# A buffer of its own for the fourth tile's rows, and its transposes ahead of half an output product

## The reference, cut to what matters

```python
def _moe2_ref(x, w_gate, w_local, w1, w2):
    logits = np.einsum('bsd,de->bse', x, w_gate)
    local_gate = 1.0 / (1.0 + np.exp(-np.einsum('bsd,de->bse', x, w_local).squeeze(-1)))
    for b in range(B):
        prev_e = -1
        for s in range(S):
            fresh_e = int(np.argmax(logits[b, s]))
            if s == 0 or local_gate[b, s] < 0.5:
                e = fresh_e
            else:
                e = prev_e if prev_e >= 0 else fresh_e
            prev_e = e
            ...                      # p = softmax(logits[b, s])
            h = np.maximum(x[b, s] @ w1[e], 0.0)     # w1[e]: 512 x 1024
            out[b, s] = p[e] * (h @ w2[e])           # w2[e]: 1024 x 512
```

## Time and profile before

| | |
|---|---|
| median of three runs | 755.41 us |
| profiled execution, its own time | 755.69 us |
| its span | 754.0 us |
| granted clock of PE, mean over the span | 0.994 |
| PE busy | 737.2 us, 98% |
| DVE, ACT, POOL busy | 299.8, 230.8, 143.0 us |
| HBM read, written | 48.79 MB, 10.31 MB |

### The profile page before, as it was taken

One profiled execution on the slowest core, in us unless ns is written; L12 is line 12 of the kernel. 1 busy time (PEld: TensorE's weight loads), 2 busy tenths in 40 slices (PEclk: granted clock), 3 DMA queues, 4 the chain that ended last, 5 costly groups with the idle time before them and its releaser, 6 DMA issues.

```text
span 754.0 us, 13862 instructions
## 1 busy us (share of the span) xinstructions
PE 737.2 (98%) x4756; PEld 672.6 (89%) x4757; DVE 299.8 (40%) x620; ACT 230.8 (31%) x435; POOL 143.0 (19%) x164
## 2 busy tenths in 40 slices
PE   6999999999999999999999999999899999999997
PEld 5879999999999999999999999888688888888885
DVE  6546241226241216241214732595534562222531
ACT  3753133114133114133113024222524462222531
POOL 7472020002020002020000015102313141211221
PEclk9999999999999999999999999999999999999999
DMA  9930314001304001300001340103832653101000
GB/s 222 384 77 15 80 30 98 1 2 49 78 27 102 1 1 45 83 15 18 1 1 37 112 157 2 57 23 105 334 114 71 216 196 110 50 28 50 30 24 12
DMA packets 71995, 57.62 MB, mean 76 GB/s; under 512 B 54892, under 2 KB 57228, under 8 KB 71952
## 3 DMA queue, kind: packets, MB, share of 16 engines
q1 hardware_dynamic: 68432, 47.58, 21.0%
q0 software_dynamic: 3520, 9.44, 3.7%
HBM read 48.79 MB, written 10.31 MB: 78 GB/s over the span
## 4 chain that ended last, share of the span: by engine, by line
PE 93%; DMA 2%; ACT 2%; DVE 1%; issue 1%; POOL 0%; SPq 0%; DVEq 0%; POOLq 0%; ACTq 0%
PE bank L606 41%; PE bank L727 15%; PE bank L752 14%; PE bank L548 4%; PE bank L577 4%; PE bank L739 2%; PE bank L519 2%; PE bank L616 2%; PE bank L571 2%; PE bank L627 2%; PE bank L675 1%; PE bank L536 1%; PE bank L558 1%; ACT wc_h L962 1%; DMA kraw<-in_k_dram 1%
## 5 line engine op out<-in xcount | busy, mean ns | idle before, releaser
L606 PE MATMUL bank<-u_h,wc_h 128*128 128x288 f32 x384 | 119.5, 311 | 0.0
L606 PE MATMUL bank<-hid_h,wc_h 128*128 128x288 f32 x384 | 117.0, 305 | 0.0
L727 PE MATMUL bank<-wslots,xgT_h 128*128 (+1 forms) x344 | 111.9, 407 | 1.6 <-DVE xgT_l L1367 1.6
L606 PE MATMUL bank<-hid_l,wc_h 128*128 128x288 f32 x384 | 113.3, 295 | 0.0
L606 PE MATMUL bank<-u_l,wc_h 128*128 128x288 f32 x384 | 113.1, 295 | 0.0
L606 PE MATMUL bank<-u_h,wc_l 128*128 128x288 f32 x384 | 113.1, 294 | 0.0
L606 PE MATMUL bank<-hid_h,wc_l 128*128 128x288 f32 x384 | 113.1, 294 | 0.0
L752 PE MATMUL bank<-wslots,hT_h 128*128 (+1 forms) x336 | 104.0, 391 | 0.0
L1376 DVE SCALAR_TENSOR_TENSOR hid_l<-bank,hid_h 128x288 fp32r<-128x288 f32 x96 | 43.4, 454 | 125.3 <-ACT hid_h L919 124.7
L919 ACT ACTIVATE hid_h<-bank 128x288 fp32r<-128x288 f32 x96 | 39.3, 409 | 117.4 <-PE bank L606 117.4
L727 PEld LDWEIGHTS bank<-wslots,xgT_h 128*128 128x128 f32 x344 | 62.0, 190 | 14.1 <-issue 2.2
(11 more groups left out here) (260 smaller groups left out, 1061.2 us busy)
## 6 DMA issues: line engine op xcount, KB each, us to landing
w1raw<-in_moe_w_dram SPq DMA_DIRECT2D x20, 512.0 KB, 3.6
w2raw<-in_moe_w_dram SPq DMA_DIRECT2D x20, 512.0 KB, 5.3
wc_raw<-in_moe_w_ch_dram SPq DMA_DIRECT2D x8, 768.0 KB, 10.1
x_rows<-x1n SPq DMA_DIRECT2D x16, 256.0 KB, 2.2
kb<-in_k_dram SPq DMA_DIRECT2D x24, 128.0 KB, 3.0
qb<-in_q_dram SPq DMA_DIRECT2D x24, 128.0 KB, 2.9
vb_e<-in_v_dram SPq DMA_DIRECT2D x16, 128.0 KB, 3.0
vb_o<-in_v_dram SPq DMA_DIRECT2D x16, 128.0 KB, 3.0
```

The source lines that it names most:

```text
L606: last = pe.matmul(to, lhsT, rhs, start=(m == 0), stop=(m == len(mms) - 1))
L727: last = pe.matmul(bank[half][:, :], xgT[a][:, c, :], w1s[x][:, bass.ds(n & 1, 1), c, half * 512:(half + 1) * 512].rearrange("p a n -> p ( ...
```

## The change

The fourth tile (tile 3) gets a row buffer `xg3`, an id buffer `id_in3` and a semaphore `x3_in` of its own. POOL clears `xg3` once, ahead of gather(0), beside the clearing of `xg`. The loop over the first three tiles in POOL's program is written out: gather(2), scatter(0), the waits for x1 and `routed` 1, gather(3) into `xg3`, a wait for `xgT_ready` 3 (that is `x_turn(2)`), gather(4) into `xg`, scatter(1), scatter(2). PE's `x_turn(3)` reads `xg3`, and stands ahead of the second six products of `output(2, 0, 0)` instead of behind them. SP waits for `x3_in` and for four gathers on `x_in`. A tensor `end_of_rows` only keeps a stretch of SBUF free, so that `xg3` lies behind it.

```diff
--- before.py
+++ after.py
@@ -181,6 +181,7 @@
             prob_t = sb(part2, "prob_t", [P, NT])
             id_in = sb(part2, "id_in", [P, 1], I32)
             id_out = sb(part2, "id_out", [P, 1], I32)
+            id_in3 = sb(part2, "id_in3", [P, 1], I32)
 
 
             table = sb(part2, "table", [1, NTP], I32)
@@ -234,6 +235,8 @@
             loads_f = sb(part2, "loads_f", [1, E])
             loads = sb(part2, "loads", [1, 2, E], I32)
             yo = sb(part2, "yo", [P, D])
+            sb(part2, "end_of_rows", [P, 1128])
+            xg3 = sb(part2, "xg3", [P, D])
 
         w1s = [wslots[:, :, x, :].rearrange("p s (c f) -> p s c f", c=KD) for x in range(2)]
         w2s = [wslots[:, :, 2 + x, :].rearrange("p s (c d) -> p s c d", c=KF) for x in range(2)]
@@ -272,7 +275,7 @@
 
         raw_in = [sem(f"raw_in{i}") for i in range(NU)]
         w_hi, w_split = sem("w_hi"), sem("w_split")
-        id_in_set, id_out_set, x_in = sem("id_in_set"), sem("id_out_set"), sem("x_in")
+        id_in_set, id_out_set, x_in, x3_in = sem("id_in_set"), sem("id_out_set"), sem("x_in"), sem("x3_in")
         rows_asked, rows_given = sem("rows_asked"), sem("rows_given")
         xgT_ready, xgT_hi, xgT_done = sem("xgT_ready"), sem("xgT_hi"), sem("xgT_done")
         h_ready, hs_done, hT_ready, hT_hi, hT_done = sem("h_ready"), sem("hs_done"), sem("hT_ready"), sem("hT_hi"), sem("hT_done")
@@ -478,7 +481,8 @@
                         load_unit(e, i)
 
             sp.wait_ge(versions_known, 1)
-            sp.wait_ge(x_in, 16 * (EARLY + 2))
+            sp.wait_ge(x3_in, 16)
+            sp.wait_ge(x_in, 16 * (EARLY + 1))
             for n in range(1, E):
                 load_weights(n)
 
@@ -670,9 +674,15 @@
                     x_turn(0)
 
             def x_turn(t):
-                pe.wait_ge(x_in, 16 * (t + 1))
+
+                of_routed = isinstance(t, int) and t == EARLY
+                if of_routed:
+                    pe.wait_ge(x3_in, 16)
+                else:
+                    pe.wait_ge(x_in, 16 * (t + 1) if isinstance(t, int) else 16 * t)
+                rows_in = xg3 if of_routed else xg
                 for c in range(KD):
-                    last = pe.transpose(bank[4][:, c * P:(c + 1) * P], xg[:, c * P:(c + 1) * P], ident[:, :])
+                    last = pe.transpose(bank[4][:, c * P:(c + 1) * P], rows_in[:, c * P:(c + 1) * P], ident[:, :])
                 last.then_inc(xgT_ready, 1)
 
             def step(name, g, n, bn, later=True):
@@ -807,8 +817,8 @@
             hidden(2, 0, 1, True)
             output(2, 0, 0, True, FIRST)
             h_turn(2, 1, True)
+            x_turn(EARLY)
             output(2, 0, 0, True, SECOND)
-            x_turn(EARLY)
             output(2, 0, 1, True, FIRST)
             pe.wait_ge(routed, 2)
             hidden(EARLY, version_of(EARLY), 0, True)
@@ -1701,14 +1711,14 @@
                 softmax_steps(n)
 
 
-            def gather(t, tokens=N):
+            def gather(t, tokens=N, rows_in=xg, id_of=id_in, landed=x_in):
                 at = ids[:, bass.ds(t, 1)]
-                pool.tensor_copy(id_in[:, :], at).then_inc(id_in_set, 1)
+                pool.tensor_copy(id_of[:, :], at).then_inc(id_in_set, 1)
                 pool.wait_ge(id_in_set, t + 1)
                 pool.sem_inc(rows_asked, 1)
-                pool.indirect_dma_start(out=xg[:, :], out_offset=None, in_=x1_rows[0:tokens, :],
-                                        in_offset=bass.IndirectOffsetOnAxis(ap=id_in[:, 0:1], axis=0),
-                                        bounds_check=tokens - 1, oob_is_err=False).then_inc(x_in, 16)
+                pool.indirect_dma_start(out=rows_in[:, :], out_offset=None, in_=x1_rows[0:tokens, :],
+                                        in_offset=bass.IndirectOffsetOnAxis(ap=id_of[:, 0:1], axis=0),
+                                        bounds_check=tokens - 1, oob_is_err=False).then_inc(landed, 16)
 
             def scatter(t, again):
                 if again:
@@ -1726,6 +1736,8 @@
             pool.wait_ge(early_ids, 1)
             pool.memset(xg[:, :], 0.0).then_inc(xg_cleared, 1)
             pool.wait_ge(xg_cleared, 1)
+            pool.memset(xg3[:, :], 0.0).then_inc(xg_cleared, 1)
+            pool.wait_ge(xg_cleared, 2)
             for stored in x1_stored:
                 pool.wait_ge(stored, 16 * ((B - 1) * HB + 1))
             gather(0, EP * J)
@@ -1742,19 +1754,26 @@
                 gather(t + 2, tokens)
                 scatter(t, again)
 
-            for t in range(EARLY):
-                if t == EARLY - 2:
-                    for stored in x1_stored:
-                        pool.wait_ge(stored, 16 * (B * HB + 1))
-                    pool.wait_ge(routed, 1)
-                tile(t, t > 0, EP * J if t < EARLY - 2 else N)
+            pool.wait_ge(xgT_ready, 2)
+            gather(2, EP * J)
+            scatter(0, False)
+
+            for stored in x1_stored:
+                pool.wait_ge(stored, 16 * (B * HB + 1))
+            pool.wait_ge(routed, 1)
+            gather(EARLY, rows_in=xg3, id_of=id_in3, landed=x3_in)
+            pool.wait_ge(xgT_ready, 3)
+            gather(EARLY + 1)
+            scatter(1, True)
+            scatter(2, True)
             pool.wait_ge(routed, 2)
             n = pool.value_load(tiles[0:1, 0:1], min_val=N // P, max_val=NT)
             with pool.Fori(EARLY, NT) as t:
                 with pool.If(t < n):
                     tile(t, True)
 
-            pool.wait_ge(x_in, 16 * n + 32)
+            pool.wait_ge(x3_in, 16)
+            pool.wait_ge(x_in, 16 * n + 16)
             pool.wait_ge(rows_stored, 16 * n)
 
     return nc
```

## The result

The changed kernel takes 750.76 us, the median of 4 runs (750.68 to 752.24), against 755.56 us (4 runs, 755.31 to 756.2) for the kernel before in the same rounds: a ratio of 0.994, interval 0.9923 to 0.9957. The forecast was 752.0, in a range of 750.6 to 754.0. The time lies inside the range, near its lower end. The profiled execution of the changed kernel took 750.76 us too, 4.93 less than the 755.69 of the one before.

A forecast was written before the change was run, and what follows sets the result against it. PE, busy 98% of the span, was taken to bound the kernel: -4.31 us in tile 3 plus 0.87 for the later hidden(3) made -3.44, so 752.0 us on the median's footing, in a range of 750.6 to 754.0.

The forecast's parts named there:

- The term that carries it: Tile 3, x_turn(4) to x_turn(5): earlier weights remove the whole stall and the clock's fall, -4.31 us.
- gather(4) and the loads: POOL and SP: gather(4) starts at 514.0 instead of 518.23, and the first w1 load also 4.2 us earlier.
- the 1.8 us that I gave the second piece to spare: Tile 3: the second w1 load lands at 524.6, while ACT wants it at 526.4.
- the 0.7 to spare behind ACT: Between h_turn and hidden: a later tile's low part is ready 0.7 us before PE needs it, so no stall.
- the wait at x_turn(3): PE idles 1.49 us for gather(3), landing at 516.45, and hidden(3) starts 0.87 late.
- the bounds of -0.29 and +0.87: Start of hidden(3): 0.29 us early if gather(3) lands at 515.26, 0.87 late if at the later landing taken.
- The sum: Whole kernel: -4.31 in tile 3 plus 0.87 at hidden(3) gives -3.44 us.
- Early landing: Rival at x_turn(3): gather(3) lands at 515.26, so -4.60 us and 750.8; chance 0.20.
- The new idle time costs the clock: Rival behind x_turn(3): the 1.49 us idle lowers PE's clock, costing 1.84 us, 753.8; chance 0.12.
- x_turn(5) waits for gather(5): Rival at x_turn(5): gather(5) comes 3 us later, PE idles nearly 2 us, 753.8; chance 0.08.
- The gathers hold each other up: Rival at x_turn(3): gather(3) lands only at 518.9, PE idles 3.9 us, +0.8, 756.2; chance 0.05.
- No effect: Rival in tile 3: the weights begin early but land as before, 755.4; chance 0.05.

The follow-up runs named there:

- e12: The kernel before, unchanged, run a third time for its trace, on a third chip: 755.9 us (1 run).
- e5: The changed kernel, with SP also waiting for the plan (`routed` 3) before it loads the weights: 753.24 us, 0.9971 of the kernel before.
- e6: The changed kernel, with SP holding the weights until hidden(3)'s first half is done: 757.09 us, 1.0019 of the kernel before.
- e7: The kernel before, with SP beginning the weights when the fourth gather has landed, not the fifth; one buffer, old order: 752.56 us, ratio 0.9969.
- e4: The changed kernel, unchanged, run again: 751.0 us, 0.9932 of the kernel before.
- e2: The kernel before, with only x_turn(3) moved ahead of the second six products, one buffer: 754.83 us, 0.9989 of the kernel before.
- e3: The changed kernel, with x_turn(3) behind the first three of the second six products: 751.77 us (6 runs).
- e8: The kernel before, unchanged, run again for its trace: 754.85 us (1 run).
- e1: The changed kernel, with x_turn(3) put back behind the second six products; own buffer and early gather stay: 750.67 us, 0.9929 of the kernel before.
- e11: The changed kernel, unchanged, run a third time: 750.81 us, 0.9936 of the kernel before.
- e9: The changed kernel, with x_turn(3) ahead of all twelve products of output(2, 0, 0): 753.69 us (1 run).
- e10: The changed kernel, with x_turn(3) behind the first three of the second six products, run again for more times: 750.8 us (6 runs).

## Why the prediction was right, and where it was off

**The term that carries it was right.** -4.31 was predicted for tile 3, and 16.61 became 12.28, -4.33. That the two meet to 0.02 is partly luck, as the first trace of before served both; against e12's tile 3 the change would be worth 5.3. e5 and e6 show that it is the weights' start and not the gather's: with every gather early and only the loads late, 2.9 and then all of it is lost. e7 shows the same from the other side.

**gather(4) and the loads** started 4.4 and 4.3 us earlier, 4.2 predicted, and there was no idle time before h_turn(3, 1). Of the 1.8 us that I gave the second piece to spare, 0.6 went because x_turn(4) came earlier than forecast, and in e4 the rest was gone too: ACT waited 0.31. That it cost nothing fits the 0.7 to spare behind ACT that the later tile showed (0.6, rather: the product behind its h_turn started 0.35 after 582.94, not 0.44). The landing itself varies: from the first load's issue to the second piece it took 5.8 to 7.1 us in the eight traces in which ACT waited for that piece (before, e2, e3, e4, e5, e6, e8, e12). The one number that I had was the short end.

**The step that was off is the wait at x_turn(3).** I took its gather to land 4.65 us after its start; x_turn(3) went on 4.2 us after it (515.25 - 511.02 and 516.55 - 512.35) in two traces of the changed kernel and 4.0 in e4. Counted as in the prediction, from where the next work would have begun (514.29, 0.35 behind h_turn's start, as before), PE stood for 0.96 us, not 1.49; the profile's bracket counts 0.71 of it. Relative to x_turn(0), x_turn(3) came 0.54 earlier than forecast, and hidden(3) 0.38 late instead of 0.87. The work between them took 3.24 us, as forecast (3.2). So the choice between the bounds of -0.29 and +0.87 was right in sign and too far out: the truth lay between, and by e1 the move costs 0.1 to 0.23 in the traces. The landing is no fixed number: with PE waiting for it, it came after 4.0 to 4.6 us in after, e2, e4, e5, e6 and e11, but after 3.5 in e9, the other bound. The reason that I gave for the late one shows again: 16 small packets make a gather, and the 16th came late. DMA packets of the changed kernel, 512.8 to 514.3 us, and then 514.3 to 514.9 us:

```profile
DMA packets 74, 0.24 MB, mean 161 GB/s; under 512 B 15, under 2 KB 15, under 8 KB 74
...
DMA packets 7, 0.02 MB, mean 41 GB/s; under 512 B 1, under 2 KB 1, under 8 KB 7
```

The 16th came past 514.3, 3.3 us after the gather's start (before: past 515.05, 3.2 after it). In e9, the landing after 3.5, all 16 small ones lie within 0.4 us:

```profile
DMA packets 26, 0.04 MB, mean 103 GB/s; under 512 B 16, under 2 KB 16, under 8 KB 26
```

The rule of the Trainium skill that a DMA counts only with all 16 increments (DMA: Bandwidth & Descriptors, "Why a DMA increments its semaphore by 16 and not by 1") fits: PE waited past the 15th. The same page's fit of 2.0 us plus bytes over 436 GB/s ("Anatomy of one DMA — SWDGE (gpsimd) path"), which made the wait vanish, does not: the estimate from it is 2.6 us for this gather, which took 3.5 at the least (e9); its neighbour took 3.45 before and 3.4 in the changed kernel. The fixed part seems not to be what is off: the changed kernel's last gather, at 735.76, moved next to no bytes and landed 2.1 us after its start (DMA packets, 735.7 to 740 us):

```profile
DMA packets 80, 0.00 MB, mean 0 GB/s; under 512 B 80, under 2 KB 80, under 8 KB 80
```

If that is the fixed part of the full gather too, its 256 KB add some 1.3 us with the queues empty (an estimate, 3.45 - 2.1), not the 0.6 of the fit.

**The sum.** At x_turn(5) -3.44 was forecast and -4.09 measured; that is 0.65 of the 1.49 by which the profiled time (750.76) missed 752.25. Another 0.72 is the low clock at 18 us in the profiled execution of before, and 0.12 are the rest. The range held, by little: the three medians of the changed kernel (750.76, 751.0, 750.81) lie 0.2 to 0.4 above its lower end. That low clock is no part of the change: it is in the traces of before, e2, e5, e7, e9, e10 and e11, and absent in those of after, e1, e3, e4, e6, e8 and e12, so in both kinds of kernel; the windows of two of them, 18 to 21.5 us, first e8 (the kernel before) and then e11 (the changed one):

```profile
18.00:21.50 3.50, 2.96 (x31) 2.71 (x30) 3.09 (x3) 3.02 (x7) 2.43 (x2) 1.00 0.93 239
```

```profile
18.00:21.50 3.50, 2.95 (x20) 2.86 (x20) 2.80 (x3) 2.92 (x7) 2.13 (x2) 0.65 0.72 212
```

On the medians the change is worth 4.8 to 5.0 us (the result, e4, e11), more than the 4.1 of the first pair of traces. Part of that is the scatter of before's tile 3, as e12 shows it: over three traces of each, x_turn(5) stands at 69.17 and 64.75, 4.4 apart. The rest, 0.4 to 0.6, is open. The kernel before also scatters more: 753.28 to 759.17 over the 17 runs beside e1 to e4, where 16 runs of the changed one stay within 2.4 us. A stall that depends on when a load lands would do that, but no trace of an execution of it near 757 or above was taken.

**The rivals.** *Early landing* had the better number, 750.8, but not for its reason: x_turn(3) came at 515.97 on the clock of before (515.25 + 0.72), halfway between its 515.35 and my 516.51, and its number meets the measured one by the 0.72 of the start, which it did not have in it. In e9 the landing was as early as it says. *The new idle time costs the clock* fell: full at 0.96 us, and at 1.81 in e9. *x_turn(5) waits for gather(5)* fell: nothing is idle before 535.29. (gather(5) did not stay where it was: at 527.48 it started 0.4 us sooner after x_turn(0) than before, as DVE wrote tile 2's output 0.8 sooner: at 523.34, where it was 524.84.) *The gathers hold each other up* fell: x_turn(3) started 4.2 us behind its gather with gather(4) behind it, and 4.56 in e2 with a scatter there. *No effect* fell with tile 3. scatter(1) slipped by 2.0, as forecast (2.2), and landed by 518.10, far ahead of the bound of 523.3.

## What to carry to other kernels

When a stall ends with a transfer, follow the chain back through the queues to the wait that let the transfer be issued: here a load of weights stood behind the landing of a gather, and taking that one wait away gave between a half and three quarters of what a buffer, a semaphore and a new order gave. Price each part by itself: the second half of this change, the transposes moved ahead, was meant to help and cost 0.1 to 0.23 us in the traces, because it put them ahead of the landing that they need; moved half as far they stood best in two traces, by 0.3 us or more, which the times did not show. And before two traces are subtracted, measure both from a common point ahead of the change, and take a second trace of the kernel before: 0.7 us of this pair came from the start, and tile 3 of the old kernel moved by 1.0 us between executions.

## What the runs showed of the hardware

- Idle time cost the clock in some traces and not in others. It fell to mostly 1.2 GHz (PEclk 0.52 to 0.54) behind these stretches ahead of hidden(4): idle 2.22 of 2.88 us in e8, 2.25 of 2.95 before, 2.26 of 2.92 in e2, 2.90 of 3.57 in e6, 3.28 of 3.94 in e12. It stayed at 2.4 GHz behind 1.96 of 2.62 in e5 and 1.81 in one piece in e9. No rule follows: 4 of the 17 runs of the kernel before beside e1 to e4 have a mean clock of 1.000, so in those it seems not to have fallen in tile 3 either, and no trace of such a run was caught.
- In e5, where it did not fall, PE still lost 0.45 us between hidden(4) and x_turn(5) (6.48 us against 6.03); with the fall it lost 1.62 before (540.10 - 532.45 = 7.65). So it seems that some 1.2 us, less than the 1.84 of the earlier trace rows, is the clock's own price.
- The fall at 18 us comes in 7 of 14 traces, and x_turn(0) then stands at 471.2 to 472.1 in place of 470.0 to 470.6: about 1.2 us, decided anew in each execution. What decides it is open.
- A gather of 128 rows landed in 3.45 us with the queues empty; gather(3) landed in 3.5 to 4.6, with another transfer 2.1 or 2.2 us behind it, and gather(4) in 6.4 under the weight loads (e7). What makes gather(3)'s 3.5 (e9) or 4.6 (e2) is open.
